# Where layer 1's square and its remainder are computed, and in which memory an attention tile is finished

## The reference, cut to what matters

```python
# attention with gates: B, H, S, D = 4, 8, 768, 40
for t in range(S):
    m_new = np.maximum(f[t] + m, i[t])
    C = exp(f[t] + m - m_new) * C + exp(i[t] - m_new) * outer(v[t], k[t])
    n = exp(f[t] + m - m_new) * n + exp(i[t] - m_new) * k[t]
    m = m_new
    y[t] = sigmoid(o[t]) * (C @ q[t]) / np.maximum(np.abs(n @ q[t]), 1.0)
x = y in rows of [B * S, 320]            # 3072 tokens
# layer 1
h = x @ w_in                             # 320 -> 2048
g = np.maximum(h, 0.0) ** 2
x = g @ w_out                            # 2048 -> 320
# layer 2, with weights of its own
h = x @ w_in2
g = np.where(h > 0.0, h, np.exp(np.minimum(h, 0.0)) - 1.0)
x = g @ w_out2
```

## Time and profile before

| | |
|---|---|
| median of 3 runs | 868.66 us (867.6 to 870.72) |
| the profiled execution | 867.17 us, its span 865.4 us |
| TensorE busy | 846.8 us, 98% of the span |
| VectorE busy | 502.6 us, 58% |
| ScalarE busy | 448.7 us, 52% |
| GpSimd busy | 388.1 us, 45% |

### The profile page before, as it was taken

One profiled execution on the slowest core, in us unless ns is written; L12 is line 12 of the kernel. 1 busy time (PEld: TensorE's weight loads), 2 busy tenths in 40 slices (PEclk: granted clock), 3 DMA queues, 4 the chain that ended last, 5 costly groups with the idle time before them and its releaser, 6 DMA issues.

```text
span 865.4 us, 15226 instructions
## 1 busy us (share of the span) xinstructions
PE 846.8 (98%) x5604; PEld 833.1 (96%) x5604; DVE 502.6 (58%) x839; ACT 448.7 (52%) x980; POOL 388.1 (45%) x422
## 2 busy tenths in 40 slices
PE   8898999999999999999999999999999999999998
PEld 7787899999999999999999999999999999999998
DVE  5587877577586675775754654444444444444443
ACT  4664565574665656656645654444444434444443
POOL 2784644454554544444524763343333333334333
PEclk9988999999999999999999999999999999999999
DMA  8663435353333453643220400000000000000000
GB/s 257 215 192 94 124 109 130 89 155 102 101 101 101 111 135 84 161 117 101 77 84 34 130 22 2 24 1 24 1 24 1 24 1 8 16 1 24 2 24 23
DMA packets 21918, 65.42 MB, mean 76 GB/s; under 512 B 3060, under 2 KB 9044, under 8 KB 19284
## 3 DMA queue, kind: packets, MB, share of 16 engines
q1 hardware_dynamic: 21268, 63.01, 25.6%
q10 hardware_dynamic: 576, 1.44, 0.5%
HBM read 57.18 MB, written 4.03 MB: 71 GB/s over the span
## 4 chain that ended last, share of the span: by engine, by line
PE 89%; DVE 5%; issue 2%; DMA 2%; POOL 1%; ACT 1%; SPq 0%; DVEq 0%; POOLq 0%
PE hps L935 40%; PE acc L949 38%; PE att L861 4%; PE att L829 2%; PE att L853 2%; PE att L866 1%; PE att L844 1%; DMA wts<-m_rows 1%; DVE glo L780 1%; DVE gate L618 1%; DVE win L693 1%; PE att L867 1%; DVE win L695 1%; POOL hact L418 0%; ACT wts L463 0%
## 5 line engine op out<-in xcount | busy, mean ns | idle before, releaser
L935 PE MATMUL hps<-xth,win 128*128 128x384 f32 x1280 | 352.6, 341 | 1.0 <-DVE hact L805 1.0
L949 PE MATMUL acc<-wout,ghi 128*128 128x320 f32 x1536 | 348.1, 313 | 0.0
L935 PE MATMUL hps<-xtl,win 128*128 128x384 f32 x768 | 260.8, 340 | 0.0
L949 PEld LDWEIGHTS acc<-wout,ghi 128*128 128x128 f32 x1536 | 258.5, 189 | 0.3 <-POOL glo L425 0.3
L949 PE MATMUL acc<-wout,glo 128*128 128x320 f32 x768 | 237.8, 310 | 0.0
L935 PEld LDWEIGHTS hps<-xth,win 128*128 128x128 f32 x1280 | 231.5, 190 | 1.6 <-issue 1.5
L425 POOL TENSOR_TENSOR glo<-hact,ghi 128x384 fp32r<-128x384 f32 x128 | 130.0, 1016 | 218.6 <-ACT ghi L593 218.5
L418 POOL TENSOR_TENSOR hact<-hact 128x384 f32<-128x384 f32 x128 | 112.7, 881 | 196.2 <-ACT hact L546 194.6
L780 DVE TENSOR_TENSOR glo<-hact,ghi 128x384 fp32r<-128x384 f32 x128 | 87.8, 686 | 134.8 <-POOL hact L418 134.0
L546 ACT ACTIVATE hact<-hps 128x384 f32<-128x384 f32 x128 | 62.6, 489 | 174.9 <-PE hps L935 174.9
L935 PEld LDWEIGHTS hps<-xtl,win 128*128 128x128 f32 x768 | 145.7, 190 | 0.0
(11 more groups left out here) (138 smaller groups left out, 724.3 us busy)
## 6 DMA issues: line engine op xcount, KB each, us to landing
raw<-in_qk SPq DMA_DIRECT2D x20, 960.0 KB, 7.1
wts<-m_rows SPq DMA_DIRECT2D x24, 512.0 KB, 4.7
kvo<-in_kvo SPq DMA_DIRECT2D x21, 484.0 KB, 7.9
x<-in_w_all SPq DMA_DIRECT2D x12, 352.0 KB, 6.3
wts<-in_w_all SPq DMA_DIRECT2D x12, 352.0 KB, 2.9
out_x<-hsum SPq DMA_DIRECT2D x16, 160.0 KB, 1.9
state_rows<-state SPq DMA_DIRECT2D x40, 52.5 KB
x<-in_w_all ACTq DMA_DIRECT2D x4, 352.0 KB, 4.9
```

Source lines behind the costliest of these rows:

```text
L935: last = nc.tensor.matmul(hps[t % 2][:, 0:NT], win[:, j, w, :], x[:, kk, :], start=(i == 0), stop=(i == len(parts) - 1))
L949: last = nc.tensor.matmul(acc[u][:, 0:DM], g[t % GR][:, cols], wout[:, j, w, :], start=(j == 0 and i == 0), stop=(j == NF - 1 and i == 2))
```

## The change

Layer 1, per step: VectorE computes the square from PSUM, `gfull = max(h, 0) * relu`, with one operand in PSUM (h) and one in SBUF (relu); GpSimd computes `glo = gfull - ghi` as in layer 2. The first product of step t now waits for VectorE's square of step t - 2. The finish of a tile writes the sum and the gated product into the PSUM bank that `within` has written, in place of SBUF; the semaphore that lets the next scores into the bank (`den_ready`) comes with x, not with the maximum. `POOL_LO` is 4, so slices 4 and 5 are split on VectorE. Tile 3's `gate_recip` stands ahead of the loop. Scores wait for each half of q's remainder apart. Four more warming products stand ahead of the first scores (the function exists already: matmuls of zeros).

```diff
-POOL_LO = 6
+POOL_LO = 4
@@ GpSimd, layer 1's step
-                        pool.wait_ge(s["relu_ready"], t + 1)
-                        wait(pool, "glo_ready", t - 1)
-                        nc.gpsimd.tensor_tensor(gfull[t % 2], relu[t % 2], relu[t % 2], ALU.mult).then_inc(s["g_ready"], 1)
+                        pool.wait_ge(s["g_ready"], t + 1)
+                        pool.wait_ge(s["ghi_ready"], t + 1)
+                        wait(pool, "g_used", T * (t - GR + 1))
+                        nc.gpsimd.tensor_tensor(glo[t % GR][:], gfull[t % 2], f32(ghi[t % GR][:]), ALU.subtract)\
+                            .then_inc(s["glo_ready"], 1)
@@ VectorE, finish(g)
-                    nc.vector.tensor_tensor(hs, hs, own, ALU.add).then_inc(s["hsum_ready"], 1)
+                    nc.vector.tensor_tensor(own, hs, own, ALU.add).then_inc(s["hsum_ready"], 1)
                     dve.wait_ge(s["hsum_ready"], with_state(g) + 1)
-                    own = hs
-                nc.vector.tensor_tensor(gt[:], gt[:], own[:, :, 0:D], ALU.mult).then_inc(s["gated_ready"], 1)
+                nc.vector.tensor_tensor(own[:, :, 0:D], gt[:], own[:, :, 0:D], ALU.mult).then_inc(s["gated_ready"], 1)
...
-                nc.vector.tensor_tensor(x1[g % 2][:, 0:DM].rearrange("t (h d) -> t h d", d=D), gt[:],
-                                        rden[:].unsqueeze(2).broadcast_to([P, H, D]), ALU.mult).then_inc(s["x_whole"], 1)
+                nc.vector.tensor_tensor(x[:, 0:DM].rearrange("t (h d) -> t h d", d=D), own[:, :, 0:D],
+                                        rden[:].unsqueeze(2).broadcast_to([P, H, D]), ALU.mult).then_inc(s["den_ready"], 1)
@@ VectorE, ahead of the loop and in layer 1's step
+            gate_recip(T)
...
-                        if g is not None:
+                        if g is not None and g > T:
                             gate_recip(g)
...
-                        dve.wait_ge(s["g_ready"], t + 1)
-                        dve.wait_ge(s["ghi_ready"], t + 1)
-                        nc.vector.tensor_tensor(glo[t % GR][:], gfull[t % 2], f32(ghi[t % GR][:]), ALU.subtract)\
-                            .then_inc(s["glo_ready"], 1)
+                        dve.wait_ge(s["relu_ready"], t + 1)
+                        wait(dve, "glo_ready", t - 1)
+                        nc.vector.scalar_tensor_tensor(out=gfull[t % 2], in0=hps[t % 2][:, 0:NT], scalar=0.0, in1=relu[t % 2],
+                                                       op0=ALU.max, op1=ALU.mult).then_inc(s["g_ready"], 1)
@@ TensorE, scores(g), the head, and first_product(t)
-                    pe.wait_ge(s["q_lo"], 2 * (with_state(g) + 1))
+                    if g >= B:
+                        pe.wait_ge(s["q_lo"], 2 * with_state(g) + u + 1)
+            keep_warm(4)
-                wait(pe, "relu_ready" if block < BLOCKS else "g_ready", t - 1)
+                wait(pe, "g_ready", t - 1)
```

More of the change, by code:

```diff
@@ L139, in mlstm_two_dense_layers @@
             "egate_ready gplus_ready gate_ready s_ps p_ready dc_ps decayed state_ready "
-            "st_hi st_lo inter_ps inter_ready intra_ps hsum_ready den_neg den_ready rden_ready gated_ready "
-            "x_whole x_ready rest_ready xt_ps xth_ready xt_ready h_ps relu_ready hneg_ready e_ready g_ready ghi_ready "
+            "st_hi st_lo inter_ps inter_ready intra_ps hsum_ready den_neg den_max den_ready rden_ready gated_ready "
+            "x_ready rest_ready xt_ps xth_ready xt_ready h_ps relu_ready hneg_ready e_ready g_ready ghi_ready "
             "glo_ready g_used acc_free win_hi win_lo win_lo_first wout_hi wout_lo out_done_0 out_done_1 out_done_2").split()
@@ L664, in finish @@
                     dve.wait_ge(s["inter_ready"], with_state(g) + 1)
-                    nc.vector.tensor_tensor(hs, hs, own, ALU.add).then_inc(s["hsum_ready"], 1)
+                    nc.vector.tensor_tensor(own, hs, own, ALU.add).then_inc(s["hsum_ready"], 1)
                     dve.wait_ge(s["hsum_ready"], with_state(g) + 1)
-                    own = hs
                 nc.vector.tensor_scalar(den[:].unsqueeze(2), own[:, :, D:E], -1.0, 1.0, ALU.mult, ALU.max).then_inc(s["den_neg"], 1)
                 dve.wait_ge(s["gate_ready"], g + 1)
-                nc.vector.tensor_tensor(gt[:], gt[:], own[:, :, 0:D], ALU.mult).then_inc(s["gated_ready"], 1)
+                nc.vector.tensor_tensor(own[:, :, 0:D], gt[:], own[:, :, 0:D], ALU.mult).then_inc(s["gated_ready"], 1)
                 dve.wait_ge(s["den_neg"], g + 1)
-                nc.vector.tensor_tensor(den[:].unsqueeze(2), den[:].unsqueeze(2), own[:, :, D:E], ALU.max).then_inc(s["den_ready"], 1)
-                dve.wait_ge(s["den_ready"], g + 1)
+                nc.vector.tensor_tensor(den[:].unsqueeze(2), den[:].unsqueeze(2), own[:, :, D:E], ALU.max).then_inc(s["den_max"], 1)
+                dve.wait_ge(s["den_max"], g + 1)
                 nc.vector.reciprocal(rden[:], den[:]).then_inc(s["rden_ready"], 1)
@@ L677, in finish @@
                 wait(dve, "xt_ps", g - 1)
-                nc.vector.tensor_tensor(x1[g % 2][:, 0:DM].rearrange("t (h d) -> t h d", d=D), gt[:],
-                                        rden[:].unsqueeze(2).broadcast_to([P, H, D]), ALU.mult).then_inc(s["x_whole"], 1)
-                dve.wait_ge(s["x_whole"], g + 1)
-                nc.vector.tensor_copy(x1[g % 2][:, DM:3 * P], x1[g % 2][:, 2 * P:DM]).then_inc(s["x_ready"], 1)
+                x = x1[g % 2]
+                nc.vector.tensor_tensor(x[:, 0:DM].rearrange("t (h d) -> t h d", d=D), own[:, :, 0:D],
+                                        rden[:].unsqueeze(2).broadcast_to([P, H, D]), ALU.mult).then_inc(s["den_ready"], 1)
+                dve.wait_ge(s["den_ready"], g + 1)
+                nc.vector.tensor_copy(x[:, DM:3 * P], x[:, 2 * P:DM]).then_inc(s["x_ready"], 1)
             def x_lo(i, par, u, bank):
```

## The result

The changed kernel takes 855.32 us (median of 4 executions, 853.78 to 857.42), the kernel before, run beside it, 868.13 us (4, 866.66 to 870.72): a ratio of 0.9851, 95% interval 0.9815 to 0.9887. Forecast were 857.5 us, 851 to 864. By the profiled executions it is 867.17 us before and 857.42 after, a gain of 9.75 us where the sum said 11.0.

What follows compares the result with a forecast made beforehand. TensorE bounds the kernel, fully busy from 110 to 460 us; 17.0 us of idle and low clock lie before. 6.0 + 3.1 + 2.4 - 0.5 = 11.0 us off gave 857.5 us; range 851 to 864.

Steps and rivals of the forecast that it cites:

- wv and the first square: Start: wv moves from 42.83 to about 40.3 us, the 1.94 us idle goes, first square over by 45.0.
- The early slow stretch: Low clock from 43.6 to 51.3 us, costing 3.4 us: may stay or go, nothing counted.
- Tile 3's x: x at 63.0 us, not 69.03; TensorE idles 1.6 us, not 5.65: 6.0 us, plus 3.1 for the slow stretch after.
- the 2.5 us added for blocked splits: VectorE before tile 3's x: 1.0 us from five longer GpSimd subtractions, 1.5 from q subtractions blocking weight splits.
- Tiles 4 and 5, +2.4 us: The finish in PSUM shortens the idles of 1.45 and 1.53 us before 92.05 and 109.58 us: 2.4 us gained.
- New waits, -0.5 us: First product now waits for VectorE's square: up to 1.5 us lost in the crowded early stretch, 0.5 taken.
- The margin of 2.5 us: Worst step from 110 us on: the square ends 2.5 us before TensorE wants the bank, so no cost.
- Free of GpSimd in PSUM: VectorE instructions with a PSUM operand, such as the square and the denominator's small ones, are not stretched by GpSimd.
- Rival 1: Backlog stays on VectorE: blocked splits put tile 3's x at 65.6 us, the clock falls, 864 us; chance 0.15.
- Rival 2: Slower: the wait on the square binds three steps after a tile's start, about 1 us a tile, 875 us; chance 0.07.
- Rival 3: Four more warming products raise TensorE's clock in the head, 17 us and more in all, 851 us; chance 0.05.
- the port rule: Two-SBUF-input VectorE instructions and SBUF-reading GpSimd ones block each other, the second to start fully; single-SBUF-input ones don't contend.

Runs made afterwards that it cites:

- Experiment 4: Changed kernel with six early splits on GpSimd again and tile 3's reciprocal back in the loop: 859.84 us, ratio 0.9921.
- experiment 2: Kernel before with only the exchange (square on VectorE, subtraction on GpSimd, first product waiting for the square): 862.58 us, ratio 0.9965.
- experiment 3: Changed kernel with the finish of a tile back in SBUF: 857.81 us, ratio 0.99.
- experiment 7: Changed kernel with a tile's finish ahead of the same step's weight split on VectorE: 855.57 us, ratio 0.9872.
- experiment 8: Finish ahead of the split, plus x's last 64 columns written from PSUM by two small products instead of an SBUF copy: 852.06 us, ratio 0.9837.
- experiment 11: Kernel of experiment 8 with TensorE's second product ahead of the transposes and scores of tiles 4 and 5: 851.01 us, ratio 0.9819.
- experiment 9: Changed kernel with one unused 2.15 us reciprocal ahead of VectorE's square, three steps after a tile's start, from step 34 on: 856.07 us, ratio 0.988.
- experiment 10: Changed kernel with two such unused reciprocals ahead of the square in those steps (15 tiles): 872.83 us, ratio 1.0068.
- experiment 1: Changed kernel with the square reading relu twice from SBUF in place of h from PSUM: 856.37 us, ratio 0.9888.
- experiment 6: Kernel before with 30 unused matmuls on TensorE just ahead of tile 3's transposes, where it idled: 865.14 us, ratio 0.999.

## Why the prediction was right, and where it wasn't

The time and the main mechanism were right: nearly all of the gain (9.0 of 9.8 us) lies ahead of 110 us, on the path wv, tile 3's x, and the slow stretch behind it. Several terms were not, and their errors partly cancelled. The terms, one by one:

- wv and the first square. wv was forecast for about 40.3 us and came at 40.74; the 1.94 us idle is 0.27; the square is over at 44.4 (forecast: by 45.0). Right.
- The early slow stretch, "I count nothing". This was too little. It is gone, and with x early nothing hides it. Experiment 4 shows the start, idle and clock together, at about 4.5 us.
- Tile 3's x at 63.0 us, with 1.6 us idle. It is done at 58.5, with no idle. The step that failed is the 2.5 us added for blocked splits: large and small splits together went down by 1.4 us. x's copy (58.35) starts 0.1 us ahead of GpSimd's q pair (58.45), which therefore blocks a split that stands behind x (2.23 us at 59.03), not one ahead of it. With so small a distance this is in part luck. So the two terms 6.0 + 3.1 = 9.1 us measure 11.6 by step 7.
- Tiles 4 and 5, +2.4 us. Wrong in sign. Tile 5's 1.53 us did go (1.7 at step 16), though not by the finish in PSUM: experiments 2 and 3 have the finish in SBUF and gain 1.7 and 1.8 us there. Tile 4's idle grew from 1.45 to 2.69 us and drew a slow stretch after it: -4.3 at step 12. Together -2.6. I had taken the finish's shorter instructions off an idle time that I held fixed, while TensorE reaches that place 11.6 us earlier and VectorE, which needs 23 us from tile 3's x to tile 4's as before, has the latter ready only 10.4 us earlier. The finish does bring tile 4's x 1 us forward (experiment 3); the slow stretch alone costs more. Experiments 7 and 8 bring the idle for x down to 0.3 and 0.5 us, and experiment 11 takes it and the fall of the clock away.
- New waits, -0.5 us. 0.3 us for the square, and 1.1 for a second wv that the prediction didn't see; both lie inside the 11.6 us above. The margin of 2.5 us fits experiments 9 and 10 (between 2.15 and 4.3).
- The sum. 11.6 - 4.3 + 1.7 = 9.0 us by step 16, and 0.8 more by step 127 that I can't place. A miss of +2.5 us by step 7 and one of -5.0 at tiles 4 and 5, 0.5 us of it taken up by the new waits' term, partly cancelled: the number was better than its parts.
- "Free of GpSimd in PSUM". Right for the square (493 to 560 ns) and for the denominator (L672 had a mean of 740 ns, L673 has 155), but by experiment 1 the square's memory is worth only 1 us or so; what carries the exchange is more likely that GpSimd now waits for the square instead of running beside VectorE's subtraction.

Rival 1 (the backlog stays) is refuted by tile 3's x at 58.5 us, but came true one tile later, at tile 4. Rival 2 (slower) is a real mechanism that stays more than 2.15 us of work a tile away. Rival 3 (TensorE warm early) is half true: the high clock in the head occurs in part of the executions, worth 1 to 3 us there and not 6. The profiled execution of after is one without it, which is part of why its 9.75 us are less than the median's 12.8: the other three, at 853.8, 853.9 and 856.7 us, have the lower mean clock (0.978 to 0.982) that marks the early rise, though they have no profile.

The copy of 64 columns was a cost that the forecast didn't see: 0.20 us alone, 1.23 us beside GpSimd, with one SBUF operand; over the 24 tiles its median rose from 195 ns before to 515 after. The prediction's reading of the port rule, that an instruction with one SBUF input doesn't contend, was too wide: it left out an exception that the section it names states, and this copy falls under it. The Trainium skill, "GPSIMD Engine Reference", section "Key points", names two kinds of VectorE instruction that contend: those with two SBUF inputs and those in a 2-port mode; and "VectorE: DVE Perf Modes", section "What auto-detection actually checks", has a single-source instruction with its source and destination in SBUF, as this copy is, run in one. The trace agrees with that (1.23 against 0.20 us), and experiment 8, where the products that read PSUM are never stretched (190 ns at most), does too.

## What to carry to other kernels

When one consumer is made early, work out its whole engine's list again for the next consumer at the new times: the idle that was small before (1.45 us here) may be small only because an earlier stall gave the late engine time to catch up (VectorE stood idle 3.93 us ahead of it before, and not at all after). Of two elementwise steps in a chain, give the one that the other engine waits for to the engine that would be disturbed: then the disturber is mostly idle while it runs (experiment 2: 3.9 us for the exchange alone). Where TensorE meets a late operand, move work that is ready ahead of the wait (experiment 11: no idle for x and an even clock, for three changed lines).

## What the runs showed of the hardware

- The length of an idle time alone didn't say whether the clock fell. It fell after 1.94 us (before, ahead of 43.6), 2.69 (after) and even 1.47 us (experiment 6), and stayed up after 2.21 us (experiment 2) and after before's 1.45 and 1.53 us. What decides between these isn't settled by these runs.
- With four matmuls more ahead of tile 0's scores, those scores took 2.05 to 2.20 us in seven of nine profiled executions and 3.78 in the other two; in the four profiles without them they took 3.78 each time. From 10 to 36 us the granted clock then reads 0.50 in the seven and 1.00 in all others, yet the speed there is the same: the 16 loads of tile 0's `within` (L861 in before) take 3.48 or 3.49 us in every profile, where such loads take 1.92 at the high clock. The 1.00 stands ahead of a trace's first recorded change, and is no guide to the speed.
- Small fp32 splits on VectorE (64 x 128, two SBUF inputs) took 0.29 us where nothing was beside them before and 0.99 to 1.00 us in after, nearly each time, since GpSimd's subtraction (1.12 us at 44.48) now starts right behind the square, and so just ahead of them (0.99 us at 44.76).
